# A fused convolution with two gated matmul layers: x loaded first, one tap on ScalarE, matmuls ahead of the first tile, and a new order in the first two chunks

## The reference

```python
out = np.einsum('hk,bskhg->bshg', softmax(weight), x_unf)       # 7 taps, 8 heads of 24
x = out.reshape(8192, 192)
gate = 1.0 / (1.0 + np.exp(-(x @ w_gate)))                      # w_gate, w_val: 192 x 1536
x1 = gate * (x @ w_val) @ w_out1                                # w_out1: 1536 x 192
h = x1 @ w_in                                                   # 192 x 2048
P = a[0] + a[1]*h + a[2]*h**2 + a[3]*h**3
Q = 1.0 + abs(b[0])*abs(h) + abs(b[1])*h**2
return (P / (Q + 1e-6)) @ w_out2                                # 2048 x 192
```

## Time and profile before

| | |
|---|---|
| median of 3 runs | 1311.41 us (1311.03 to 1311.74) |
| the profiled execution, device time | 1310.99 us |
| its span in the trace | 1309.2 us |
| granted TensorE clock, mean | 0.99 |
| TensorE matmul busy | 1259.6 us, 5440 matmuls |
| VectorE busy | 1252.4 us |
| ScalarE busy | 1105.6 us |
| GpSimd busy | 658.4 us |
| first matmul | 15.92 us after the span's start |
| table load on ScalarE | 1.28 us each |
| gate product on VectorE, mean in the first chunk | 0.68 us |

### The profile page before, as it was taken

How to read it: one execution, slowest core, us unless ns; L and a number is a source line. 1 busy time by engine, 2 the same in 40 slices (tenths; PEclk the granted TensorE clock), 3 DMA queues, 4 the chain that set the end, 5 groups by cost and what they waited for, 6 DMA issues and landing times.

```text
span 1309.2 us, 16870 instructions
## 1 busy us (share of the span) xinstructions
PE 1259.6 (96%) x5440; PEld 1022.5 (78%) x5440; DVE 1252.4 (96%) x1201; ACT 1105.6 (84%) x1278; POOL 658.4 (50%) x337
## 2 busy tenths in 40 slices
PE   5989999999999999999999999999999999999866
PEld 4868888788888888888887888878888888888654
DVE  7779999999999999999999999999999999989998
ACT  6579888888988888898988888888898888888773
POOL 1425555455556456456455455555455545554433
PEclk9989999999999999999999999999999999999898
DMA  8000000000000000000000100000000000000000
GB/s 225 25 1 21 2 13 21 9 25 0 25 7 12 20 5 27 0 12 20 8 24 0 32 0 12 20 8 24 0 21 12 12 20 0 20 1 13 1 13 12
DMA packets 15960, 23.66 MB, mean 18 GB/s; under 512 B 2240, under 2 KB 10048, under 8 KB 15936
## 3 DMA queue, kind: packets, MB, share of 16 engines
q1 hardware_dynamic: 14160, 21.30, 5.7%
q10 hardware_dynamic: 1776, 2.06, 0.7%
HBM read 13.13 MB, written 6.29 MB: 15 GB/s over the span
## 4 chain that ended last, share of the span: by engine, by line
PE 87%; DVE 8%; issue 3%; ACT 1%; POOL 1%; DMA 0%; SPq 0%; DVEq 0%; POOLq 0%; ACTq 0%
PE up_ps L304 11%; PE up_ps L305 10%; PE up_ps L306 10%; PE up_ps L307 10%; PE up_ps L308 10%; PE acc_main L311 7%; PE acc_main L312 7%; PE acc_main L314 7%; PE acc_tail L313 7%; PE acc_tail L315 7%; DVE denom L1201 1%; DVE numer L1164 1%; DVE denom L1191 1%; DVE denom L1154 1%; DVE numer L1172 1%
## 5 line engine op out<-in xcount | busy, mean ns | idle before, releaser
L983 POOL TENSOR_TENSOR frac_low<-denom,seed 128x1024 fp32r<-128x1024 f32 x126 | 377.3, 2994 | 526.9 <-DVE denom L1201 524.9
L974 POOL TENSOR_TENSOR gated_low<-gated,gated_high 128x512 fp32r<-128x512 f32 x192 | 264.1, 1392 | 109.6 <-ACT gated_high L658 109.6
L304 PE MATMUL up_ps<-x_high,up_high 128*128 128x512 f32 x640 | 254.8, 398 | 34.6 <-DVE x_low L1233 15.9
L305 PE MATMUL up_ps<-x_high,up_low 128*128 128x512 f32 x640 | 251.7, 393 | 0.0
L306 PE MATMUL up_ps<-x_low,up_high 128*128 128x512 f32 x640 | 251.4, 393 | 0.0
L307 PE MATMUL up_ps<-x_tail_high,up_tail 128*128 128x512 f32 x640 | 251.0, 392 | 0.0
L308 PE MATMUL up_ps<-x_tail_low,up_tail 128*128 128x512 f32 x640 | 250.8, 392 | 0.0
L678 ACT ACTIVATE numer<-up_ps,coef 128x1024 f32<-128x1024 f32 x128 | 154.4, 1206 | 34.2 <-PE up_ps L308 30.7
L1164 DVE TENSOR_TENSOR numer<-up_ps,numer 128x1024 f32<-128x1024 f32 x128 | 156.2, 1220 | 24.6 <-ACT seed L669 18.6
L669 ACT ACTIVATE seed<-up_ps,coef 128x1024 f32<-128x1024 f32 x128 | 142.6, 1114 | 41.3 <-PE up_ps L308 27.9
L304 PEld LDWEIGHTS up_ps<-x_high,up_high 128*128 128x128 f32 x640 | 121.5, 190 | 69.5 <-DVE denom L1154 21.4
(11 more groups left out here) (87 smaller groups left out, 2254.7 us busy)
## 6 DMA issues: line engine op xcount, KB each, us to landing
x_raw<-x_chunks SPq DMA_DIRECT2D x16, 393.0 KB, 3.1
out_chunks<-out_main SPq DMA_DIRECT2D x16, 256.0 KB, 2.1
tail_twice<-conv SPq DMA_DIRECT2D x60, 64.0 KB, 2.0
out_chunks<-tail_part SPq DMA_DIRECT2D x16, 128.0 KB, 2.3
numer<-w_out SPq DMA_DIRECT2D x1, 1536.0 KB, 8.5
seed<-w_out ACTq DMA_DIRECT2D x1, 1152.0 KB, 14.5
denom<-w_in SPq DMA_DIRECT2D x2, 512.0 KB, 4.7
denom<-w_gate SPq DMA_DIRECT2D x1, 576.0 KB, 5.8
```

The lines of the kernel that those rows point to most:

```text
L304: nc.tensor.matmul(acc, up_high[:, cols], x["high"][:], start=True, stop=False)
L305: nc.tensor.matmul(acc, up_low[:, cols], x["high"][:], start=False, stop=False)
L974: nc.gpsimd.tensor_tensor(gated_low[:, b], gated[:, b], gated_high[:, b], ALU.subtract).then_inc(gated_low_done, 1)
L983: nc.gpsimd.tensor_tensor(ring(frac_low, j, 2, LOW_RING), ring(denom, j), ring(seed, j), ALU.mult).then_inc(frac_low_done, 1)
```

## The change

Semaphores: the two small loads get one each. SyncE loads x first, then gate 0, coef, val 0, gate 1; ScalarE's queue loads the logits as its first instruction. ScalarE makes tap 0 of chunk 0's main blocks, between exp and abs. VectorE makes taps 1 to 6 of it, splits gate 0 before x0's tail, and waits for abs ahead of val 0's split. TensorE multiplies 16 times 128x384 of the rounded gate 0 by itself into acc2_tail, which nobody reads, once gate 0's main part is rounded and the tail block's conv is done. The first up tile's five matmuls each wait for their own operands, with x0's low part last. The lists of chunks 0 and 1 are put in another order; the loop's body isn't changed.

```diff
-            sp.dma_start(logits[:], conv_logits).then_inc(small_in, 16)
-            sp.dma_start(coef[:], rational_coef).then_inc(small_in, 16)
             sp.dma_start(x_raw[:], x_chunks[0]...).then_inc(x_in, 16)
...
             load_piece(sp, "gate", 0)
+            sp.dma_start(coef[:], rational_coef).then_inc(coef_in, 16)
             load_piece(sp, "val", 0)
...
+            def warm_up():
+                pe.wait_ge(w_high_done, 1)
+                pe.wait_ge(conv0_tail_step, taps)
+                for _ in range(WARM_UPS):                      # WARM_UPS = 16
+                    nc.tensor.matmul(acc2_tail[:, 0:G_TILES * P], up_high[:, 0:P], up_high[:, 0:G_TILES * P],
+                                     start=True, stop=True)
+            def up_first():
+                acc, cols = up_bank(0, 0, GATE_PLACES[0]), slice(0, P)
+                pe.wait_ge(w_high_done, 2)
+                pe.wait_ge(x0_main_high, 1)
+                nc.tensor.matmul(acc, up_high[:, cols], x0["high"][:], start=True, stop=False)
+                pe.wait_ge(w_low_done, 1)
+                nc.tensor.matmul(acc, up_low[:, cols], x0["high"][:], start=False, stop=False)
+                pe.wait_ge(w_low_done, 2)
+                pe.wait_ge(x0_tail_high, 1)
+                nc.tensor.matmul(acc, up_tail[:, cols], x0["tail_high"][:], start=False, stop=False)
+                pe.wait_ge(x0_tail_low, 1)
+                nc.tensor.matmul(acc, up_tail[:, cols], x0["tail_low"][:], start=False, stop=False)
+                pe.wait_ge(x0_main_low, 1)
+                nc.tensor.matmul(acc, up_high[:, cols], x0["low"][:], start=False, stop=True).then_inc(gate_ready, 1)
...
             up_val(0, 1, 1)
+            up_val(0, 1, 2)
             down_gated(0, 0, 0)
-            up_val(0, 1, 2)
             down_gated(0, 0, 1)
+            down_gated(0, 0, 2)
             up_gate(0, 2, 0)
-            down_gated(0, 0, 2)
...
             down_gated(1, 0, 0)
+            down_gated(1, 0, 1)
             up_gate(1, 1, 0)
...
             up_h(1, 2, 1)
-            down_gated(1, 0, 1)
             down_gated(1, 0, 2)
+            down_fraction(1, 1, 0)
             down_gated(1, 1, 0)
             down_gated(1, 1, 1)
-            down_gated(1, 1, 2)
             up_gate(1, 2, 0)
...
-            act.wait_ge(small_in, 32)
-            nc.scalar.activation(abs_b[:], coef[:, 4:6], ACT.Abs).then_inc(soft_act, 1)
+            act.dma_start(logits[:], conv_logits).then_inc(logits_in, 16)
             act.wait_ge(soft_dve, 2)
             nc.scalar.activation(tap_w[:], logits[:], ACT.Exp).then_inc(soft_act, 1)
+            act.wait_ge(x_in, 16)
+            act.wait_ge(soft_dve, 6)
+            nc.scalar.activation(conv[:, 0:BLOCKS - 1], x_raw[:, 0:BLOCKS - 1, 0:HALF], ACT.Identity,
+                                 scale=tap_w[:, 0:1]).then_inc(conv_step, 1)
+            act.wait_ge(coef_in, 16)
+            nc.scalar.activation(abs_b[:], coef[:, 4:6], ACT.Abs).then_inc(soft_act, 1)
...
             sigmoid(0, 0, 0)
+            round_weights_main("val", 1)
+            round_weights_tail("val", 1)
             sigmoid(0, 0, 1)
-            round_weights_main("val", 1)
             sigmoid(0, 0, 2)
-            round_weights_tail("val", 1)
+            round_weights_main("out1", 0)
             round_gated(0, 0, 0)
-            round_weights_main("out1", 0)
+            sigmoid(0, 1, 0)
             round_gated(0, 0, 1)
             round_weights_tail("out1", 0)
             round_weights_main("in", 0)
-            sigmoid(0, 1, 0)
             sigmoid(0, 1, 1)
             round_gated(0, 0, 2)
+            round_gated(0, 1, 0)
             sigmoid(0, 1, 2)
...
-            split_x0_tail(0)
             split_weights("gate", 0)
+            split_x0_tail(0)
...
             split_weights_main("val", 1)
+            split_weights_tail("val", 1)
             gate(0, 0, 0)
-            split_weights_tail("val", 1)
...
             sum_x1_tail(1)
+            split_weights_tail("out2", 0)
+            split_x1_tail(1)
+            split_x1_main(1)
             gate(1, 0, 0)
-            split_x1_main(1)
-            split_x1_tail(1)
...
             product(1, 1, 0)
+            rest(1, 1, 0)
             quadratic(1, 2, 0)
```

125 lines of the change are left out of this document (64 added, 61 removed).

## The result

The changed kernel takes 1313.04 us (median of 21 runs, 1310.86 to 1314.22); the kernel before, measured beside it, 1311.19 us (21 runs, 1309.44 to 1312.20). The ratio is 1.0013, 95% interval 1.0007 to 1.0018: slower by 0.13%, inside what I called no change, but on the other side of zero and above the range of 1304.8 to 1311.6. The means differ by 1.66 us (1312.60 against 1310.94, 0.6 uncertain at 95%), and I go by means where two kernels lie within 2 us. The profiled execution took 1311.43 us, 0.44 more than the one before. It is one of the faster runs of the change, so the two traces show less than the loss.

The account below looks back on a forecast made before the run. TensorE's unbroken matmuls bound the kernel, so time could be won only where it stands or runs at half clock: 2.35 us head start at 62 plus 1.4 at the stall, 3.75 in all, median 1307.7 us, range 1304.8 to 1311.6.

Parts of the forecast that it names:

- Part 1: Start of the convolution: x issued earlier, first tap at about 4.15 us; gain 0.75, bounds 0.9 and -0.3.
- wrong in the first step: The prediction's own sign of failure at the front: tile 2 starting after 16 us.
- Rival E: At the front: logits land after x, conv starts at 4.9 or later; 1308.2 us, chance 0.12 together with rival B.
- Part 2: First main tap moved to ScalarE: takes 0.51 us off VectorE's chain at the start.
- Part 3: First up tile: passes run as operands come, only x0's low part waits for VectorE's splits; gain 1.88 us.
- Part 4: Sixteen matmuls ahead raise the clock, so six slow passes after tile 1 become fast; about 1.0 us.
- Rival B: After tile 1: matmuls ahead don't keep the clock up, ten slow passes remain; 1308.1 us, chance 0.12 together with rival E.
- What gives part of it back: TensorE waits 1.6 us at the twelfth tile for the fifth sigmoid, 1.8 with smaller losses; head start at 62: 2.35.
- The stall after x1: From about 72.5 to 94 us: a down tile in the stall and fewer slow passes; 1.4 us, bounds -1.5 and +2.5.
- Rival D: At about 92 us TensorE stands at the first low fraction, rest landing 6.4 us late; 1314.5 us, chance 0.10.
- In the loop nothing is changed: Loop: VectorE has 1.3 us to spare per chunk and can follow an earlier TensorE; 0, at worst -1.1 us.
- C: Rival: no wait at the twelfth tile, only 0.2 us of loss; 5.15 or more gained, 1305.5 us, chance 0.10.

Follow-up runs that it names:

- e1: The changed kernel's new front with every list from the first sigmoid on as in the kernel before; 1309.40 us, ratio 0.9992 to the kernel before.
- e17: The changed kernel with 12 added matmuls ahead of the first tile instead of 16; 1311.96 us, ratio 1.0007 to the kernel before.
- e2: The old front of the kernel before with the changed kernel's new lists of chunks 0 and 1; 1310.65 us, ratio 0.9996 to the kernel before.
- e5: The changed kernel with the old lists of chunk 1 on all four engines; 1310.84 us, ratio 0.9996 to the kernel before.
- e6: The changed kernel with chunk 1's old lists and the logits as SyncE's first transfer; 1310.22 us, ratio 0.9990 to the kernel before.
- e8: The changed kernel with ScalarE's slope and magnitude ahead of the rounding of x0's tail, in chunk 2 alone; 1309.31 us, ratio 0.9987 to the kernel before.
- e10: The changed kernel with chunk 2's slope and magnitude ahead of the tail's rounding and the logits ahead of x on SyncE; 1308.22 us, ratio 0.9982.

## Why the prediction was wrong

**Part 1, start of the convolution: wrong, with the sign.** The term was +0.75, from "if the logits land near 2.5"; its lower bound of -0.3 had them at 3.4. They landed at 4.12, and the term measures -0.80; tile 2 started at 16.54, past the 16 that the prediction gave as its own sign of being wrong in the first step. The bound was worked out from x's stream; the nearest row for a small load on a queue beside a large one I didn't have, and should have taken x's own landing (3.1 to 3.2 us) as what a load beside x can take. The Trainium skill (DMA: Bandwidth & Descriptors, Queues, rings and completion order) says that a DMA engine takes turns between queue rows, a packet at a time; the trace agrees in so far as the logits' 144 packets on their own queue took 3.37 us beside x's and 1.7 ahead of them, but does not show the turns. Rival E had this at the front (logits behind x, which landed at 3.92; conv at 4.9 or later), and the sigmoid's wait did shrink, as it said; its time of 1308.2 failed on the same later step as the forecast.

**Part 2 and Part 3: right.** From first tap to tile 1's last pass it is now 16.20 - 5.69 = 10.51 us, before 17.80 - 4.89 = 12.91: 2.40 saved, where 0.51 + 1.88 = 2.39 was the sum.

**Part 4: right.** 1.0 forecast, 2.73 - 1.60 = 1.13 measured. The matmuls ran from 9.31 rather than 7.5, and delayed nothing: tile 1 was released by x0's high part, 0.44 us after them. Rival B is out.

**What gives part of it back: the right place, a smaller size.** Forecast 1.6 at the twelfth tile by the fifth sigmoid. In the change this tile stands 0.84 longer than a pass (28.04 to 29.11); the view names VectorE's split, which ends at 29.08, but the sigmoid that its bank waits for ended at 28.97, and e1, where the old order leaves it the last by far, has it as the releaser. With 2.73 of head start and not 4.15 TensorE came 1.4 later by that, so there was less to wait. Two small waits at 54.4 and 56.2, which I said weren't there, take 0.7. Head start at 62: 0.98 for 2.35. Part 1 alone takes 1.55; the sigmoid's smaller wait and Part 4 give back a little more than the two small waits take.

**The stall after x1: right in the profiled run, not in every run.** TensorE's timeline of the changed kernel:

```profile
74.72 0.80 PE L311 MATMUL acc_main<-gated_high,down 128*128 128x512 f32 x1 [3.03 <-POOL gated_low L1007]
...
77.02 0.63 PE L304 MATMUL up_ps<-x_high,up_high 128*128 128x512 f32 x1
...
78.20 0.39 PE L307 MATMUL up_ps<-x_tail_high,up_tail 128*128 128x512 f32 x1
```

One down tile alone in the stall at half the clock, then the gates at 77.02, and two or three slow passes of theirs for ten: from 0.64 to 3.28 is 2.64 won, forecast 1.7; the wait before the first low fraction is 0.2 longer than the old one, forecast 0.3. That is one faster run of the change against a slower one of the kernel before. In e17 the clock stays down, and 1.4 us of it are gone: the term "1.0 won of slow clock" came true in these profiles by luck as much as by the mechanism, and I gave the clock a bound upward only. That rival B (matmuls ahead don't keep the clock up) was about the wrong place: the clock was lost after the second idle stretch, not after the first. Rival D had its place right, but its wait was 1.1 us and not over 6.

**"In the loop nothing is changed ... 0, at worst -1.1": this step failed**, and turned the result. I went from the stall straight to the loop's steady state and used VectorE's spare time there as the slack of the way in. The 40 us between, chunk 1's last window and the first tiles of chunk 2, I never followed on ScalarE and VectorE, though the change exchanges many places in them. The runs show in its place -3.4 us (0.84, 0.34 and 2.25): two low parts that now come late, and a denominator with 0.5 us to spare, delayed by a later tap, a slower copy, the order on ScalarE and a split that takes 0.94 longer. The two low parts belong to chunk 1's new order: e2 has both waits with the old front, and e5 and e6 have neither. e8, which undoes the order on ScalarE alone, gives back 2.4 us of marker and 3.25 of mean (2.2 against the change's own lower group, whose mean was 1311.5).

Two sums of the rivals don't come out as written: C names 0.2 us of loss and takes 0.4 off, and its 5.15 alone gives 1306.3; D's 3.75 and 2.6 give 1314.0, not 1314.5. Nothing in the outcome hangs on either.

With the front and the entry mended (e10) the marker is 2.56 ahead of the kernel before and the mean 2.5, for a forecast of 3.75; the waits at 54 to 56, 113 and 128 us are still there.

## What to carry to other kernels

A head start arrives only if every chain that it has to pass comes earlier with it. A chain that doesn't, or that the change itself makes later, has only its slack: before crediting a head start to the end time, find at the entry of each stage what was the last operand to come, by how much it was early, and which of its inputs the early engine doesn't feed. Don't take the average spare time of the loop for it. An in-order engine's list is part of such a chain: an instruction that waits for a DMA should stand behind those that feed the bound engine. And where two halves of a change lose nothing singly and lose together, look for the wait in which one's earliness meets the other's lateness.
